# Attention and two mixing layers on one core: input weights by output halves, and the second batch's spatial weights turned on VectorE

## What is computed

```python
# 1. attention; every query sees n_local = 96 keys behind it and n_global = 8 first keys, with a slope bias
scores = q @ k.T / sqrt(D) + bias;  a = softmax(scores where kept);  x = a @ v      # [B, 768, 512]
# 2. gated mixing over positions
h = relu(x @ w_in)                          # 512 -> 1024
u, v = h[..., :512], h[..., 512:]
v_n = (v - mean(v)) / sqrt(var(v) + 1e-6)
v_s = w_spatial @ v_n + b_spatial[:, None]  # 768 x 768 over positions
x = (u * v_s) @ w_out
# 3. low rank over positions (rank 32), then a channel MLP
u = x + (x.T @ U @ V).T
out = u + relu(u @ w_ch1) @ w_ch2           # 512 -> 2048 -> 512
```

## Time and profile before

| what | value |
|---|---|
| median of 3 runs | 559.49 us (557.4 to 560.1) |
| the profiled execution | 562.82 us, of which the span of the trace is 560.7 us |
| TensorE busy with matmuls | 533.7 us, 95% |
| VectorE busy | 289.5 us, 52% |
| ScalarE busy | 174.3 us, 31% |
| GpSimd busy | 112.0 us, 20% |
| mean granted TensorE clock | 0.98 |

### The profile page before, as it was taken

One profiled execution on the slowest core, in us unless ns is written; L12 is line 12 of the kernel. 1 busy time (PEld: TensorE's weight loads), 2 busy tenths in 40 slices (PEclk: granted clock), 3 DMA queues, 4 the chain that ended last, 5 costly groups with the idle time before them and its releaser, 6 DMA issues.

```text
span 560.7 us, 7652 instructions
## 1 busy us (share of the span) xinstructions
PE 533.7 (95%) x2728; PEld 418.3 (75%) x2728; DVE 289.5 (52%) x845; ACT 174.3 (31%) x429; POOL 112.0 (20%) x134
## 2 busy tenths in 40 slices
PE   7688999899999999999989999999999999999996
PEld 5455666567777788878768888888888888888884
DVE  5748888857775534689822265523146524011012
ACT  4755665645555533332311101021010102101010
POOL 5884000000000001498389500000000000000000
PEclk8969999989999999999989999999999999999999
DMA  7975454545514000055223100002000002000002
GB/s 179 226 158 130 102 102 105 119 97 130 122 47 129 29 30 0 2 168 161 84 76 112 39 0 1 0 1 75 1 0 2 0 2 75 1 0 1 0 1 79
DMA packets 45835, 36.25 MB, mean 65 GB/s; under 512 B 29504, under 2 KB 39744, under 8 KB 45792
## 3 DMA queue, kind: packets, MB, share of 16 engines
q1 hardware_dynamic: 39776, 19.34, 15.6%
q0 software_dynamic: 3216, 11.63, 6.9%
q10 hardware_dynamic: 2800, 4.72, 2.9%
HBM read 32.54 MB, written 3.15 MB: 64 GB/s over the span
## 4 chain that ended last, share of the span: by engine, by line
PE 80%; DVE 10%; POOL 4%; issue 3%; DMA 2%; ACT 1%; DVEq 0%; POOLq 0%; ACTq 0%
PE ps L1255 66%; PE ps L1228 5%; PE ps L1299 4%; PE ps L1272 4%; DVE uT_first L1051 2%; DMA w_raw<-in_moe_w_in 2%; POOL win_lo L464 2%; DVE pr L923 1%; PE ps L1390 1%; POOL win_hi L462 1%; DVE uT_lo L1058 1%; DVE wspT_lo L1010 1%; DVE sc L907 1%; DVE gv_lo L991 1%; POOL small L486 0%
## 5 line engine op out<-in xcount | busy, mean ns | idle before, releaser
L1176 DVE SCALAR_TENSOR_TENSOR hT_lo<-ps,hT_hi 128x512 fp32r<-128x512 f32 x48 | 33.2, 692 | 171.4 <-ACT hT_hi L773 171.4
L773 ACT ACTIVATE hT_hi<-ps 128x512 fp32r<-128x512 f32 x48 | 28.8, 599 | 228.2 <-PE ps L1255 228.2
L597 ACT ACTIVATE pr<-sc,small 128x256 f32<-128x256 f32 (+1 forms) x96 | 46.2, 483 | 52.2 <-DVE small L907 46.8
L907 DVE CUSTOM_DVE_ANT_0 sc<-ps,bias 128x256 f32<-128x256 f32 (+1 forms) x96 | 35.0, 400 | 22.8 <-PE ps L1272 21.2
L1255 PE MATMUL ps<-win_hi,xT_hi 128*128 128x512 f32 x96 | 40.9, 427 | 0.0
L1051 DVE STREAM_TRANSPOSE ys<-tokens 32x128 f32<-32x128 f32 x128 | 38.7, 302 | 1.8
L1255 PE MATMUL ps<-uT_hi,w1a_hi 128*128 128x512 f32 x96 | 38.0, 396 | 1.0 <-DVE uT_lo L1058 1.0
L1255 PE MATMUL ps<-win_hi,xT_lo 128*128 128x512 f32 x96 | 38.5, 401 | 0.0
L1255 PE MATMUL ps<-win_lo,xT_hi 128*128 128x512 f32 x96 | 38.4, 400 | 0.0
L1255 PE MATMUL ps<-uT_lo,w1a_hi 128*128 128x512 f32 x96 | 38.1, 397 | 0.0
L1255 PE MATMUL ps<-uT_hi,w1a_lo 128*128 128x512 f32 x96 | 38.0, 396 | 0.0
(11 more groups left out here) (154 smaller groups left out, 1096.4 us busy)
## 6 DMA issues: line engine op xcount, KB each, us to landing
w_raw<-in_moe_w_ch POOLq DMA_DIRECT2D x16, 512.0 KB, 4.0
wsp<-in_moe_w_spatial ACTq DMA_DIRECT2D x12, 384.0 KB, 3.7
vn<-in_v SPq DMA_DIRECT2D x12, 256.0 KB, 3.7
out<-ys SPq DMA_DIRECT2D x12, 256.0 KB, 2.2
qk_late<-in_q SPq DMA_DIRECT2D x24, 112.0 KB, 3.5
qk_late<-in_k SPq DMA_DIRECT2D x24, 112.0 KB, 3.7
vp<-in_v SPq DMA_DIRECT2D x10, 224.0 KB, 4.5
w_raw<-in_moe_w_in POOLq DMA_DIRECT2D x4, 512.0 KB, 6.0
```

Of the source, the lines that this page charges most:

```text
L597: act.activation(pr[:, k % 3, e, 0:w], sc[:, k % 2, e, 0:w], ACT.Exp, bias=nmax[:, k % 2, e:e + 1], scale=-1.0, accum_out=sums[:, k % 3, e ...
L773: act.activation(hT[0][:, n % 2, :], h1_ps(n), ACT.Relu).then_inc(s["hT_hi"], 1)
L907: dve.tensor_tensor_reduce(out=sc[:, k % 2, e, 0:w], in0=scores_ps(k, e)[:, 0:w], in1=bias[:, 2 * p + e, WINDOW - w:WINDOW], scale=-SCALE, ...
L1176: dve.scalar_tensor_tensor(hT[1][:, n % 2, :], h1_ps(n), 0.0, hT[0][:, n % 2, :], ALU.max, ALU.subtract).then_inc(s["hT_lo"], 1)
```

## The change

- **Input weights.** A chunk of `w_in` is now 256 rows of one output half: V's half first (two chunks), then U's. TensorE waits for chunk q + 1 at piece q of the first tile, and starts one unit sooner (`LAG` = 6, `ALONE` = 30), so 18 units are left for stage 2. The wait for `xT_lo` moves behind the unit's transposes. VectorE's layer norm steps move one unit up: `statistics` now stands in the unit with `turn_next`, `normed` in the one with `x_lo`.
- **U and V** are loaded on SP's queue at tile 4, and split by GpSimd after the deviation of tile 3; ScalarE's part stands at unit 20. GpSimd's `deviation` steps stand between the chunks of `w_out`.
- **Banks.** The attention output alternates between two banks for tiles 6 and 7 too (`PAIRED` = 8).
- **Spatial weights of batch 1.** TensorE transposes none of them. ScalarE's queue loads them with four DMAs a tile, in pieces of 32 columns (`load_blocks`), so that a transpose by VectorE in 32x32 blocks gives the whole transpose (`turn_wsp`, two instructions of 128x384 a tile). `wsp_hi` and `wsp_lo` read the result from SBUF. There are two buffers, and tiles 0 and 1 are made in stage 3.
- **Tokens for the first MLP block.** VectorE turns a tile with one instruction of 128x512 into `u_rows` (`turn_rows`), and SP moves the blocks to their places in `uT_first` with 16 DMAs of 16 KB. `u_rows` is one buffer: `turn_rows(n)` waits until the 16 moves of tile n - 1 have landed. It stands in VectorE's stage 3, after the layer norms of tiles 2 to 5. MLP blocks 2 and 3 are turned as before.
- **Entry order.** For batch 1 the last two tiles make V, V, U, U (`u_v_late`). `hidden(0)`, the first MLP step, stands before the last but one `low_rank` and the last `project`.

The core of the diff; the memory layout, the branch that doesn't run and lines that repeat are left out:

```diff
@@ -48,9 +48,10 @@
-LAG = 7
+LAG = 6
...
+PAIRED = (ALONE + NP) // NP
...
@@ -251,7 +269,7 @@
-            return ps[:, 6 + (tile % 2 if tile < NT else 0), :]
+            return ps[:, 6 + (tile % 2 if tile < PAIRED else 0), :]
...
@@ -376,7 +403,9 @@
             if name == "in":
-                return w_in[c * P:(c + 1) * P, :], [w[:, c, :] for w in win]
+                at, n = c % 2 * 2, slice((1 - c // 2) * DM, (2 - c // 2) * DM)
+                return (w_in[at * P:(at + 2) * P, n].rearrange("(a p) n -> p a n", p=P),
+                        [w[:, at:at + 2, n] for w in win])
             if name == "ch1":
...
@@ -418,10 +447,17 @@
                     sp.wait_ge(s["k_loaded1"], 16)
-                if tile == 2:
+                if tile == 4:
+                    sp.dma_start(u_raw, U.rearrange("(k p) r -> p k r", p=P)).then_inc(s["u_loaded"], 16)
                     for a in range(P // RANK):
...
                 load_v(tile)
+            for n in range(TB):
+                sp.wait_ge(s["u_blocks"], n + 1)
+                for x in range(TURNS):
+                    for y in range(TURNS):
+                        sp.dma_start(uT_first[y * TURN:(y + 1) * TURN, :, n * P + x * TURN:n * P + (x + 1) * TURN],
+                                     u_rows[x * TURN:(x + 1) * TURN, :, y, :]).then_inc(s["u_moved"], 16)
             for m in range(B * NT):
...
@@ -510,10 +545,11 @@
                     split_piece(n, r)
-                if n == 0:
-                    pool.dma_start(u_raw, U.rearrange("(k p) r -> p k r", p=P)).then_inc(s["u_loaded"], 16)
+                if n >= ready["in"] - 1:
+                    deviation(n - ready["in"] + 1)
+            deviation(3)
             split_u_v()
-            for m in range(NT):
+            for m in range(4, NT):
                 deviation(m)
...
@@ -580,6 +616,12 @@
+            def load_blocks(t):
+                if t < NT:
+                    for y in range(TURNS):
+                        act.dma_start(wsp_blocks(t)[y * TURN:(y + 1) * TURN, :, :, :].rearrange("p a k c -> p (a k) c"),
+                                      blocks_d[t, y, :, :, :]).then_inc(s[f"blocks_loaded{t % 2}"], 16)
...
@@ -652,12 +694,22 @@
                     gv_hi(b, t - 1)
-                u_relu(b, t, wide)
+                if t == NT - 1:
+                    gv_hi(b, t)
+                    u_relu(b, t - 1, wide)
+                if t != NT - 2:
+                    u_relu(b, t, wide)
             def wsp_hi(b, t, h, wide):
-                wait(act, "wsp_transposed", b * (2 * NT) + 2 * t + h + 1)
-                act.activation(wspT[0][:, h * HALF:(h + 1) * HALF, :].rearrange("p k n -> p (k n)"),
-                               wsp_ps(h, wide), ACT.Copy).then_inc(s["wspT_hi"], 1)
+                half = slice(h * HALF, (h + 1) * HALF)
+                if b:
+                    act.wait_ge(s["wsp_turned"], 2 * t + h + 1)
+                    src = wsp_turned[t % 2][:, half, :].rearrange("p k n -> p (k n)")
+                else:
+                    wait(act, "wsp_transposed", 2 * t + h + 1)
+                    src = wsp_ps(h, wide)
+                act.activation(wspT_of(b, t)[0][:, half, :].rearrange("p k n -> p (k n)"), src,
+                               ACT.Copy).then_inc(s["wspT_hi"], 1)
...
@@ -753,19 +822,28 @@
                     probs_out(a + 1)
-                    wsp_hi(after, (t + 1) % NT, 0, False)
+                    if t + 1 < NT:
+                        wsp_hi(0, t + 1, 0, False)
                     exps(a + 4)
-                    wsp_hi(after, (t + 1) % NT, 1, False)
-                    load_wsp((t + 2) % NT)
+                    if t + 1 < NT:
+                        wsp_hi(0, t + 1, 1, False)
+                    if t + 2 < NT:
+                        load_wsp(t + 2)
+                    elif t + 2 == NT:
+                        load_blocks(0)
                     if a + 2 <= LAST:
...
                 x2_hi(0, NT - 1, False)
+                load_blocks(1)
                 relus(1, 0, True)
...
                     relus(1, t, True)
-                gv_hi(1, NT - 1)
+                    if t <= 2:
+                        for h in range(2):
+                            wsp_hi(1, t - 1, h, True)
+                        load_blocks(t + 1)
...
@@ -1004,10 +1082,24 @@
+            def turn_wsp(t):
+                dve.wait_ge(s[f"blocks_loaded{t % 2}"], 16 * TURNS * (t // 2 + 1))
+                if t % 2 == 0:
+                    dve.wait_ge(s["mixed"], NT + max(t - 1, 0))
+                elif t > 1:
+                    dve.wait_ge(s["mixed"], NT + t - 1)
+                for h in range(2):
+                    half = slice(h * HALF, (h + 1) * HALF)
+                    dve.transpose(wsp_turned[t % 2][:, half, :].rearrange("p k (r a) -> p a k r", a=TURNS),
+                                  wsp_blocks(t)[:, :, half, :]).then_inc(s["wsp_turned"], 1)
...
                 dve.wait_ge(s["wspT_hi"], b * (2 * NT) + 2 * t + h + 1)
-                hi, lo = [w[:, h * HALF:(h + 1) * HALF, :].rearrange("p k n -> p (k n)") for w in wspT]
-                dve.tensor_tensor(lo, wsp_ps(h, wide), hi, ALU.subtract).then_inc(s["wspT_lo"], 1)
+                half = slice(h * HALF, (h + 1) * HALF)
+                hi, lo = [w[:, half, :].rearrange("p k n -> p (k n)") for w in wspT_of(b, t)]
+                src = wsp_turned[t % 2][:, half, :].rearrange("p k n -> p (k n)") if b else wsp_ps(h, wide)
+                dve.tensor_tensor(lo, src, hi, ALU.subtract).then_inc(s["wspT_lo"], 1)
...
@@ -1039,6 +1131,13 @@
+            def turn_rows(n):
+                wait(dve, "u_ready", n + 1)
+                dve.wait_ge(s["u_moved"], 16 * TURNS * TURNS * n)
+                dve.transpose(u_rows[:, :, :, :].rearrange("p c y r -> p (c y) r"),
+                              tokens[:, n, :].rearrange("p (m r) -> p m r", r=TURN)).then_inc(s["u_blocks"], 1)
...
@@ -1061,20 +1160,19 @@
                     gate(b, t, True)
-                    for h in range(2):
-                        if t + 1 < NT:
+                    if b and t + 2 < NT:
+                        turn_wsp(t + 2)
+                    if b == 0 and t + 1 < NT:
+                        for h in range(2):
                             wsp_lo(b, t + 1, h, True)
-                    for x in range(2):
-                        if b and t < TB:
-                            turn_tokens(t, x)
+                    if b and 0 < t <= TB:
+                        uT_lo(0, t - 1)
                     if t:
...
                     gT_lo(b, t)
-                    for x in range(2, TURNS):
-                        if b and t < TB:
-                            turn_tokens(t, x)
-                    if b and t >= 2:
-                        uT_lo(0, t - 2)
+                    for h in range(2):
+                        if b and t + 2 < NT:
+                            wsp_lo(b, t + 2, h, True)
...
@@ -1155,20 +1258,29 @@
                     turn_next(a + 1)
-                    wsp_lo(after, (t + 1) % NT, 0, False)
+                    if t + 1 < NT:
+                        wsp_lo(0, t + 1, 0, False)
                     if a + 2 <= LAST:
...
                         turn_next(a + 2)
-                    wsp_lo(after, (t + 1) % NT, 1, False)
+                    if t + 1 < NT:
+                        wsp_lo(0, t + 1, 1, False)
                 x_lo(TILES - 1)
...
                 for t in range(1, NT):
+                    if t <= 2:
+                        turn_wsp(t - 1)
                     if t <= 3:
...
                     layer_norm(1, t)
+                    if 2 <= t:
+                        turn_rows(t - 2)
+                    if 2 <= t <= 3:
+                        for h in range(2):
+                            wsp_lo(1, t - 2, h, True)
                 gv_lo(1, NT - 1)
...
@@ -1291,7 +1403,7 @@
                     pe.wait_ge(s[f"v_loaded{buf}"], 16 * values_loaded(tile))
-                    wait(pe, "xT_lo", tile if tile > NT else tile - 1)
+                    wait(pe, "xT_lo", tile if tile > PAIRED else tile - 1)
                 values = [vp, vn] if tile % NT else [vn]
...
@@ -1354,6 +1466,16 @@
+            def u_v_late(b, t, wide):
+                for q in (0, 1):
+                    u_v_piece(b, t, q, wide)
+                for q in (2, 3):
+                    if t == NT - 1:
+                        u_v_piece(b, t - 1, q, wide)
+                for q in (2, 3):
+                    if t != NT - 2:
+                        u_v_piece(b, t, q, wide)
...
@@ -1441,7 +1564,12 @@
                     if between is not None:
-                        u_v_piece(0, between // NP, between % NP, False)
+                        t, q = between // NP, between % NP
+                        if t == 0:
+                            pe.wait_ge(s["chunk_split"], q + 1)
+                        if q == 0:
+                            wait(pe, "xT_lo", t + 1)
+                        u_v_piece(0, t, q, False)
```

(68 more changed lines are left out.)

60 lines of the change are left out of this document (32 added, 28 removed).

## The result

| | before | after |
|---|---|---|
| median | 559.24 us (4 runs) | 580.45 us (4 runs) |
| ratio, 95% interval | | 1.038 (1.0355 to 1.0406) |
| profiled execution, its span | 562.82, 560.7 us | 578.98, 577.0 us |
| TensorE busy | 533.7 us, 95% | 529.0 us, 92% |
| mean granted clock | 0.98 | 0.973 |

The forecast was 563.5 us, with a range of 544 to 572. The kernel is slower, as forecast, but the time lies outside the range.

A forecast was written before the change was run, and what follows sets the result against it. TensorE, busy 95% of the span, was taken to bound the kernel. Front -6.7 plus stages 3 and 4 +10.7 gave +4.0 us, from a 559.5 median to 563.5, range 544 to 572.

The forecast's parts named there:

- front, stages 1 and 2: Stages 1 and 2 together, from sooner input pieces to the extra unit: -6.7 us, between -3 and -9.
- stages 3 and 4 without the moves: Stages 3 and 4: fewer TensorE transposes and waits gone, against a lost cover and a longer VectorE and ScalarE chain.
- the moves, with the clock behind them: Stages 3 and 4: moves at 8.8 us a tile delay the last gv_lo, +14.2 us; low clock afterwards +2.8.
- my upper bound of 0.56: SP's queue: dearest issue considered for a move, 0.56 us, from V's piece there; it gives 10.7 us a tile.
- The layer norm: Stage 1, steps one unit up: VectorE about 0.3 us behind TensorE's need in five tiles, +1.5 us (0 to +3).
- The collision: Stage 1, unit 10: VectorE's normalisations beside GpSimd's split of U and V, which moves to unit 20 to 22: -1.0 us.
- the sooner pieces: Stage 1: the first input piece comes at unit 6, at about 28.4 instead of 33.35 us: -4.9 us.
- the second bank: Stage 1, tile 7: the wait of 1.96 us and the low clock behind it go, -3.3 us (-2 to -3.6).
- One more unit in stage 2: Stage 2: an additional unit without an input piece costs +1.7 us.
- Rival 3: Stage 4: VectorE's wsp_lo, both inputs in SBUF, slows beside GpSimd's splits; slower still, 568.5 us; chance 0.14.
- Rival 4: Stage 1: the front gains nothing, as another load or VectorE holds unit 6 to 9; 567.5 us; chance 0.06.
- the main case: Whole kernel: 563.5 us, its own range 558 to 570, chance 0.50.

The follow-up runs named there:

- f1: The kernel before with only the change's front part (weight halves, late U and V, LAG 6, PAIRED), stages 3 and 4 as before: 560.52 us, ratio 1.002.
- e1: The kernel after with 1 of each tile's 16 moves, the other blocks zeros: 557.78 us, ratio to the kernel before 0.9958.
- e2: The kernel after with all 16 moves a tile, each one run of 128 bytes a partition (4 KB instead of 16): 576.56 us, ratio 1.031.
- f2: f1 with the layer norm steps of stage 1 in the units where they stood before the change: 553.57 us, ratio 0.990.
- e4: The kernel after with the layer norm steps of stage 1 back in the units they had before the change: 580.79 us, ratio 1.0371.
- h2: A second profile of e4's kernel, unchanged: that run took 575.38 us.
- h1: The kernel after with turns of x spread over stages 3 and 4, layer norm steps back, ScalarE's block loads later: 548.76 us, ratio 0.9799.
- g4: The kernel after with 8 of each tile's 16 moves issued by SP and 8 by ScalarE: 575.22 us, ratio 1.0275.

## Why the forecast was wrong

The runs part the change into three. Forecast and measured, in us (measured by ratios, times 559.3):

| part | forecast | measured | from |
|---|---|---|---|
| front, stages 1 and 2 | -6.7 | +1.1 | f1 |
| stages 3 and 4 without the moves (and block loads in stage 2) | -7.4 | -3.5 | e1 less f1 |
| the moves, with the clock behind them | +18.1 | +23.6 | after less e1 |
| sum | +4.0 | +21.2 | |

- **The moves: right mechanism, size too small.** That `turn_rows` waits for the moves, that the layer norms and the last `gv_lo` stand behind it, and that each us of a tile's moves counts three, all came as written. The step that failed is "15 x 0.432 + 2.2 + 0.1 = 8.8 us a tile". It took its issue from a load with the same shape from memory. Inside SBUF the same shape takes 0.601 + 0.04, outside my upper bound of 0.56. 15 x 0.64 + 1.9 = 11.5; in the first tile one issue took 1.40. No run shows why a move inside SBUF is dearer to issue than a load, only that neither bytes nor runs make it so (e2). Turn to turn is 12.3 to 13.2 instead of 9.9, so TensorE idles 23.5 us instead of 15.3. A turn itself takes 0.71, not 1.11. The clock cost an estimated 4 us instead of 2.8: TensorE worked again from 261.3 us on, at 0.50 until 268 and at 0.82 until 272.
- **The layer norm: the failed step of the front.** I gave its new place +1.5, from the order of the steps. It is worth 6.7, give or take 2 (f2 against f1): TensorE waits 0.75 and 0.80 us at units 10 and 14 and 2.41 at unit 22, and in some executions the clock falls to half behind that last wait. I had priced the sum of work in the unit, not that VectorE's normalisation then meets GpSimd's split, with nothing left between VectorE and TensorE to take it up.
- **The collision was only moved.** I took -1.0 between 0 and -2.0. It was gone at unit 10, where 0.76 us of 2.02 is left, and came back at unit 22 with 2.41: no gain. With the layer norm back, 0.72 us of it is left (f2).
- **Right in the front**: the sooner pieces (unit 10 at 43.13 instead of 47.76, -4.6 of the forecast -4.9 - 1.0) and the second bank (the 1.96 us are gone). One more unit in stage 2 was +1.7; stage 2 of f1 is 83.1 us, +2.0.
- **Left out: ScalarE's queue in stage 2.** I priced `load_blocks` in stage 4 and removed 0.7 for the transposes in stage 2, but not its first four issues, which stand ahead of attention's last units. Their issue is 0.667 us, not 0.43, and ScalarE stands still meanwhile; stage 2 is 1.7 longer than f1's. With the layer norm back it is 3.7 longer (e4 and h2 against f2's 84.1), with half clock behind.
- **Rival 3** holds as a mechanism: the spatial low halves, both inputs in SBUF, take up to 4.5 us a pair beside GpSimd's splits and 1.0 alone. In the kernel after they took 1.54 or less, since VectorE reached most of them late, so next to nothing of it reached the time. Where the long wait is gone it does: 1.04 us of TensorE behind a pair of 3.49 in e1, 3.54 us behind a pair of 3.49 and a move in h1. By the Trainium skill (SBUF — State Buffer, Who interferes with whom) a VectorE instruction with two SBUF inputs contends with GpSimd's reads, and one with a single SBUF input doesn't, outside VectorE's two-port modes. The traces agree: the turns of the spatial weights, with one input, took 1.54 to 1.61 a pair with GpSimd or without.
- **Rival 4**, that the front gains nothing, came true in its outcome and not in its mechanism. Units 6 to 9 weren't held (29.23, 32.40, 35.61 and 38.82 us in the kernel after); the gain went at units 10, 14 and 22 and in stage 2. It stood at 0.06.
- **The range** was drawn around the main case and each rival by itself. What fell outside is their sum: two misses of the same sign, in the moves and in the front. My terms came from one execution, and the bounds of the issue only from rows of loads.

Open: f1's profiles start the first mixing product at 113.3 and 117.1, the kernel before at 119.4 and 118.0, and f1 loses 2.0 in stage 2. That is -1.5 by the means, against a measured +1.1 (-0.2 to +2.4). I found no wait for the difference; the clock in stage 4 moves by more from run to run. Whether `u_rows` with two buffers would do as well as spreading wasn't tried.

## What to carry to other kernels

Before a stage is handed to a DMA queue, count the issues: here each small DMA inside SBUF cost its queue 0.6 us, with 4 KB or with 16, and ScalarE did nothing else while it issued them. Look at what stands behind the wait for them in the waiting engine's order: spreading the same 64 moves gave back 18 us without touching one of them. And when a software pipeline is shifted by one step, look again at what was dealt over its steps: here, leaving the layer norm where it had been was worth more than the step.

## What the runs showed of the hardware

- An issue on SP's or ScalarE's queue that moves 32 partitions inside SBUF takes 0.59 to 0.62 us in the median, on SP's for 4 KB and 16 KB alike (after, e2); two queues issue side by side at nearly the same pace (0.602 and 0.623, g4).
- The same wait of 2.41 us is followed by full clock in one execution and by half clock in another (f1, g2), with an identical program. A profile shows one of them; f1's was 3.7 us below its median.
- A transpose by VectorE of 128x512 took 0.71 us, where the earlier trace rows has 1.11 for the same size with other layouts of input and output.
